# Gate logits of five dense chunks on VectorE instead of TensorE

## The reference

```python
attn = softmax(q k^T / 8, masked to 4 sink columns and a window of 128) v     # 4 x 8 heads, 768 rows, 64 wide
x = attn as (3072, 512)
h = x @ w_in                                # 512 -> 2048
y = (h * cos(h)) @ w_out                    # 2048 -> 512: the dense layer
logits = y @ w_gate + modality_bias[modality_id]      # (3072, 8)
e_idx = argmax(logits, axis=1)
gate_w = softmax(logits)[row, e_idx]
out[row] = gate_w * (relu(y[row] @ w1[e]) @ w2[e])    # e = e_idx[row]
```

## Time and profile before

| What | Value |
|---|---|
| device time, median of 3 runs | 1204.62 us (1203.62 to 1204.96) |
| span of the profiled execution | 1203.8 us |
| TensorE matmul busy | 1145.4 us (95%), 6588 instructions |
| VectorE busy | 618.9 us (51%), 1522 instructions |
| ScalarE busy | 493.6 us (41%), 1099 instructions |
| GpSimd busy | 86.7 us (7%) |
| chain that ended last | PE 86%, DVE 4%, issue 3%, DMA 3%, ACT 1% |

### The profile page before, as it was taken

The page is one execution under the profiler, slowest core; times in us unless marked ns, Lnnn a source line. Parts: engine busy times, 40 slices in busy tenths (PEclk is TensorE's granted clock), DMA queues, the critical chain, the costliest instruction groups (busy, mean ns, idle before and its releaser), DMA issues.

```text
span 1203.8 us, 20823 instructions
## 1 busy us (share of the span) xinstructions
PE 1145.4 (95%) x6588; PEld 961.5 (80%) x6589; DVE 618.9 (51%) x1522; ACT 493.6 (41%) x1099; POOL 86.7 (7%) x174
## 2 busy tenths in 40 slices
PE   6999999989999999999999999997599999999996
PEld 5777777768888888888888888886589999899895
DVE  7888888854454444444345445445773222252221
ACT  5777777753333333333334334332352221241221
POOL 0000000000000000000000000000111121221121
PEclk9999999989999999999999999998599999999998
DMA  5444444510001002002002000000573111121110
GB/s 118 143 142 142 142 142 142 173 67 1 1 9 63 1 0 70 0 0 70 0 0 70 0 0 36 1 1 35 193 257 111 35 52 36 36 105 52 35 50 18
DMA packets 33993, 76.61 MB, mean 64 GB/s; under 512 B 10398, under 2 KB 10398, under 8 KB 33952
## 3 DMA queue, kind: packets, MB, share of 16 engines
q1 hardware_dynamic: 29312, 63.50, 17.1%
q0 software_dynamic: 4640, 12.59, 3.1%
HBM read 58.77 MB, written 19.92 MB: 65 GB/s over the span
## 4 chain that ended last, share of the span: by engine, by line
PE 86%; DVE 4%; issue 3%; DMA 3%; SPq 2%; ACT 1%; POOL 0%; DVEq 0%; POOLq 0%; ACTq 0%
PE bank L1310 23%; PE bank L1324 22%; PE bank L1450 14%; PE bank L1438 12%; PE bank L1185 4%; DMA v_sink<-v_n 3%; PE bank L1219 2%; PE bank L1230 2%; PE bank L1197 2%; PE bank L1342 1%; PE bank L1420 1%; SPq L403 1%; PE bank L1411 1%; SPq L395 1%; PE bank L1187 1%
## 5 line engine op out<-in xcount | busy, mean ns | idle before, releaser
L1310 PE MATMUL bank<-x_hi,w_hi 128*128 128x512 f32 x384 | 156.1, 406 | 4.7 <-issue 4.2
L1310 PE MATMUL bank<-x_lo,w_hi 128*128 128x512 f32 x384 | 153.0, 399 | 0.0
L1310 PE MATMUL bank<-x_hi,w_lo 128*128 128x512 f32 x384 | 152.7, 398 | 0.0
L1324 PE MATMUL bank<-w_hi,g_hi 128*128 128x512 f32 x384 | 152.3, 397 | 0.4 <-DVE g_lo L986 0.4
L1324 PE MATMUL bank<-w_hi,g_lo 128*128 128x512 f32 x384 | 152.1, 396 | 0.0
L1324 PE MATMUL bank<-w_lo,g_hi 128*128 128x512 f32 x384 | 151.8, 395 | 0.0
L1145 DVE SCALAR_TENSOR_TENSOR h_lo<-bank,h_hi 128x256 fp32r<-128x256 f32 x112 | 47.6, 425 | 173.4 <-ACT h_hi L756 172.2
L1450 PE MATMUL bank<-xg_hi,w_hi 128*128 128x256 f32 x448 | 127.7, 285 | 4.3 <-DVE xg_lo L1139 2.8
L974 DVE TENSOR_SCALAR whole<-turns 128x512 f32<-128x512 f32 x96 | 41.0, 427 | 175.4 <-ACT turns L707 175.4
L1185 PE MATMUL bank<-k_sb,qz 128*128 128x256 f32 (+1 forms) x384 | 114.7, 400 | 16.8 <-DMA v_sink<-v_n 16.8
L707 ACT ACTIVATE turns<-bank 128x512 f32<-128x512 f32 x96 | 57.5, 599 | 177.7 <-PE bank L1310 177.7
(11 more groups left out here) (159 smaller groups left out, 2087.8 us busy)
## 6 DMA issues: line engine op xcount, KB each, us to landing
raw<-w_expert SPq DMA_DIRECT2D x32, 512.0 KB, 4.9
raw<-w_dense SPq DMA_DIRECT2D x16, 512.0 KB, 4.5
k_sb<-k_t SPq DMA_DIRECT2D x16, 384.0 KB, 3.3
qz<-q_t SPq DMA_DIRECT2D x32, 192.0 KB, 4.0
v_sb<-v_n SPq DMA_DIRECT2D x16, 384.0 KB, 4.4
xT_scratch<-x_stage SPq DMA_DIRECT2D x16, 384.0 KB, 4.6
x_raw<-xT_scratch SPq DMA_DIRECT2D x6, 1024.0 KB, 5.1
y_scratch<-y_sb SPq DMA_DIRECT2D x6, 1024.0 KB, 4.3
```

The lines of the kernel that those rows point to most:

```text
L1310: last = pe.matmul(H_BANK[f % 2][:, :], a[:, w], b[:, k, :], start=x == 0, stop=x == 3 * KD - 1)
L1324: last = pe.matmul(Y_BANK[t][:, :], a[f % 4][:, t * P:(t + 1) * P], b[:, w], start=f == 0 and x == 0, stop=f == FB1 - 1 and x == 2)
```

## The change

Five of the six chunks no longer send y through TensorE for their logits. The gate matrix is loaded once, transposed and flat, into all 128 partitions (`gate_rows`, 8 rows of 512 in the buffer `raw`, 2 MB in SBUF), by one DMA on SyncE's queue after `load_chunk(1)`. VectorE then makes each logit column of a tile with one `tensor_tensor_reduce`: it multiplies a tile of `y_sb` with one gate row and sums along the row. That is 4 tiles x 8 experts = 32 of them for each chunk, three in each of steps 1 to 10 of the next chunk and two in step 11: after `frac`, after `g_sb` and after `g_lo`. The product itself goes to `whole`, which is not used, so each waits for the one before. `turns`, `frac` and `cosine` become one tile. In the last four steps of the last chunk `choose_early` does the routing operations for the first 20 tiles, and after the last chunk they run over 4 tiles only. The last chunk's own turns and products are as before.

```diff
             turns = sb("turns", [P, CH], where=a)
             whole = sb("whole", [P, CH], where=a)
-            frac = sb("frac", [P, CH], where=a)
-            cosine = sb("cosine", [P, CH], where=a)
+            frac = cosine = turns
...
-        yT_sb = raw[:, 3, 0:D]
+        gate_rows = raw[:, :, :].rearrange("p a b -> p (a b)").rearrange("p (e d) -> p e d", e=NE)
...
+            load_chunk(1)
+            sp.wait_ge(w_lo_made, 2 * PIECES)
+            sp.dma_start(raw[:, :, :].rearrange("p a b -> p (a b)"), w_gate_rows.partition_broadcast(P)).then_inc(gate_rows_loaded, 16)
+            store_chunk(0)
-            with sp.Fori(1, NCH) as c:
+            with sp.Fori(2, NCH) as c:
...
-            def turn_y(c, t):
-                act.wait_ge(y_turned, CT * c + t + 1)
-                act.activation(yT_sb[:, :], TURN_BANK[:, :], ACT.Copy).then_inc(yT_made, 1)
             def copy_y(c):
                 act.wait_ge(down_done, FB1 * (c + 1))
                 act.wait_ge(y_sb_free, c + 1)
+                at_least(act, early_logits, CT * NE * c)
...
-                    if not first and f in (5, 7, 9, 11):
-                        turn_y(c - 1, (f - 5) // 2)
                     act.wait_ge(hidden_done, n + 1)
-                    at_least(act, frac_made, n)
+                    at_least(act, g_made, n)
...
+            def early_logit(c, i):
+                t, e = i // NE, i % NE
+                if i == 0:
+                    dve.wait_ge(gate_rows_loaded, 16)
...
+                at_least(dve, early_logits, CT * NE * c + i)
+                dve.tensor_tensor_reduce(out=dump[:, :], in0=y_sb[:, t, :], in1=gate_rows[:, e, :], scale=1.0, scalar=0.0,
+                                         op0=ALU.mult, op1=ALU.add,
+                                         accum_out=sums_of[:, CT * c + t, e:e + 1]).then_inc(early_logits, 1)
+            def some_logits(c, f, part):
+                i = 3 * (f - 1) + part
+                if c > 0 and 0 <= i < CT * NE:
+                    early_logit(c - 1, i)
...
+                    dve.wait_ge(frac_made, n + 1)
+                    some_logits(c, f, 0)
                     dve.wait_ge(cos_made, n + 1)
                     at_least(dve, g_lo_made, n)
                     dve.tensor_tensor(g_sb[:, :], H_BANK[f % 2][:, :], cosine[:, :], ALU.mult).then_inc(g_made, 1)
...
+                    some_logits(c, f, 1)
                     dve.wait_ge(g_hi_made, n + 1)
                     dve.tensor_tensor(g_lo[f % 4][:, :], g_sb[:, :], g_hi[f % 4][:, :].bitcast(F32), ALU.subtract).then_inc(g_lo_made, 1)
+                    some_logits(c, f, 2)
...
+                    if c == NCH - 1 and f >= FB1 - 4:
+                        choose_early(f - FB1 + 4)
...
-            with dve.Fori(1, NCH - 1) as c:
-                dense(c)
-            dense(NCH - 1, split_next=False)
+            for c in range(1, NCH):
+                dense(c, split_next=c < NCH - 1)
...
-            dve.wait_ge(logits_done, NT)
-            after(link(dve.tensor_tensor(logits[:, :, :], L_BANK[:, 0:NT * NE].rearrange("p (t e) -> p t e", e=NE),
-                                         bsel, ALU.add)))
+            late = slice(EARLY, NT)
+            few = [P, CT, NE]
+            dve.wait_ge(logits_done, CT)
+            after(link(dve.tensor_tensor(logits[:, late, :], L_BANK[:, 0:CT * NE].rearrange("p (t e) -> p t e", e=NE),
+                                         bsel[:, late, :], ALU.add)))
...
-                    if not first and f in (4, 6, 8, 10):
-                        turn_y(c - 1, (f - 4) // 2)
-                    if not first and f in (5, 7, 9, 11):
-                        route(c - 1, (f - 5) // 2)
```

More of the change, by code:

```diff
@@ L1008, in _, with choose_early @@
             full = [P, NT, NE]
+            EARLY = NT - CT
+            def choose_early(part):
+                at = slice(0, EARLY)
+                shape = [P, EARLY, NE]
+                if part == 0:
+                    dve.wait_ge(early_logits, CT * NE * (NCH - 1))
+                    after(link(dve.tensor_tensor(logits[:, at, :], sums_of[:, at, :], bsel[:, at, :], ALU.add)))
+                    link(dve.tensor_reduce(top[:, at], logits[:, at, :], AX.X, ALU.max))
+                elif part == 1:
+                    after(made[0])
+                    link(dve.tensor_tensor(weighed[:, at, :], logits[:, at, :], wide(top[:, at], shape), ALU.is_equal))
+                    link(dve.tensor_tensor(tmp[:, at, :], logits[:, at, :], wide(top[:, at], shape), ALU.subtract))
+                elif part == 2:
+                    after(made[0])
+                    after(link(dve.tensor_tensor(weighed[:, at, :], weighed[:, at, :],
+                                                 down[:, :].unsqueeze(1).broadcast_to(shape), ALU.mult)))
+                    link(dve.tensor_reduce(first_max[:, at], weighed[:, at, :], AX.X, ALU.max))
+                else:
+                    after(made[0])
+                    link(dve.tensor_tensor(onehot[:, at, :], weighed[:, at, :], wide(first_max[:, at], shape), ALU.is_equal))
+            dense(0)
             dve.wait_ge(const_loaded, 48)
@@ L1016, in _ @@
             after(n)
-            for m, x in enumerate((bsel, bpart)):
+            for m, x in enumerate((bsel[:, :, :], bpart[:, :, :])):
                 n = link(dve.tensor_tensor(x, bias_sb[:, m:m + 1, :].broadcast_to(full), wide(is_mod[:, m, :], full), ALU.mult))
             after(n)
-            after(link(dve.tensor_tensor(bsel, bsel, bpart, ALU.add)))
-            with dve.Fori(1, NCH - 1) as c:
-                dense(c)
-            dense(NCH - 1, split_next=False)
+            after(link(dve.tensor_tensor(bsel[:, :, :], bsel[:, :, :], bpart[:, :, :], ALU.add)))
+            for c in range(1, NCH):
+                dense(c, split_next=c < NCH - 1)
             dve.wait_ge(y_sb_free, NCH)
@@ L1327, in down @@
                 return last
-            def turn_y(c, t):
-                if t < 2:
-                    pe.wait_ge(y_copied_act, 2 * c + t + 1)
-                else:
-                    pe.wait_ge(y_copied_dve, 2 * c + t - 1)
-                for k in range(KD):
-                    last = pe.transpose(TURN_BANK[:, k * P:(k + 1) * P], y_sb[:, t, k * P:(k + 1) * P], ident[:, :])
-                last.then_inc(y_turned, 1)
-            def route(c, t):
-                pe.wait_ge(yT_made, CT * c + t + 1)
-                at = (CT * c + t) * NE
-                for k in range(KD):
-                    last = pe.matmul(L_BANK[:, bass.ds(at, NE)], yT_sb[:, k * P:(k + 1) * P], wg_sb[:, k, :],
-                                     start=k == 0, stop=k == KD - 1)
-                last.then_inc(logits_done, 1)
             def dense(c, last_chunk=False):
```

57 lines of the change are left out of this document (33 added, 24 removed).

## The result

| | before | changed |
|---|---|---|
| device time, median | 1204.29 us (1203.62 to 1204.96, 4 runs) | 1176.60 us (1176.14 to 1178.19, 4 runs) |
| ratio | | 0.9767 [0.9747, 0.9786] |
| span of the profiled execution | 1203.8 us | 1175.1 us |
| TensorE matmuls | x6588, 1145.4 us | x6348, 1118.3 us |
| VectorE busy | 618.9 us | 720.3 us |

2.3% faster: 1176.6 us against a forecast of 1176.8. The profiled execution itself took 1176.95 us.

The account below looks back on a forecast made before the run. TensorE, never idle in the dense layer, was taken as the bound. Removing turns and products (26.6 us) and shortening routing (1.2 us) gave 27.8 us off the 1203.8 us span, forecasting a 1176.8 us median, range 1173.5 to 1182 us.

Parts of the forecast that it names:

- TensorE's term, 26.6 us: Dense layer: removing turns (0.44 us) and products (0.89 us), 20 pairs, saves 26.6 us, at least 23.4.
- The reduce, x = 0.70 us: VectorE, dense layer: one 512-element reduce takes 0.70 us, making its step 4.6 us against TensorE's 5.6.
- Its place: Two of three reduces lie in VectorE's 0.70 us waits for ScalarE, the third in idle time behind `g_lo`; cost 0.
- Beyond it each chunk loses 31x - 34.0: Dense layer: with reduce time x over 1.10 us, `hidden` waits for `g_sb`, losing 31x - 34.0 us a chunk.
- x = 1.10 us: Dense layer: the reduce time beyond which TensorE's `hidden(13)` would wait for VectorE's `g_sb` of step 11.
- ScalarE, the DMA, the seven early operations: 0 each: ScalarE's lost copies and new wait, the 2 MB gate-row load, and `choose_early` each cost 0 on the path.
- Routing, 1.2 us: After the last chunk: seven VectorE operations on 32 instead of 192 elements save 1.2 us, bounds 0 and 1.2.
- The clock, 0 and 2.5 to either side: Behind routing: TensorE's rise from half clock may shift; taken as 0, with 2.5 us either side.
- The sum: Whole kernel: 26.6 + 1.2 = 27.8 us off the 1203.8 us span, plus 0.8 to the median, gives 1176.8 us.
- 1: Dense-layer reduces run at half rate with both sources in SBUF, x = 1.22 us; 1195.9 us; chance 0.06.
- 2: Dense-layer reduces cost two full passes, x = 1.40 us, making VectorE the bound; 1223.8 us; chance 0.03.
- 3: Dense layer: no gain, as large matmuls slow beside reduces or another wait fills the gaps; about 1204 us; chance 0.02.

Follow-up runs that it names:

- each half by itself: Changed kernel with the transposes of y, or the products with w_gate, put back on TensorE, results unused: 1188.66 us and 1198.54 us.
- all three behind `g_lo`: Changed kernel with all three reduces of a step moved behind `g_lo`, none where VectorE waits for ScalarE: 1196.61 us.
- free fourth reduce: Changed kernel with one extra reduce, result unused, in each step that has reduces: 1176.63 us.
- 5 and 6 reduces: Changed kernel with two or three extra reduces, results unused, in each step that has reduces: 1184.16 us and 1221.71 us.
- kernels of old order: The ten traced kernels with attention first in TensorE's first branch, general path behind it; their 384th large matmul starts from 352.26 to 354.19 us.
- either form: Changed kernel's reduces, or the 160 rewritten as scalar_tensor_tensor with an accumulator; the rewritten kernel took 1177.98 us.
- the exchange: Changed kernel with the sides of TensorE's first branch swapped, unused general path first, attention last: 1173.91 us.

## Why the prediction was right

- **TensorE's term, 26.6 us.** Right: 5.29 us a chunk by the windows, 26.4 for the five, and each half by itself 1.74 and 3.52 us a chunk against 1.76 and 3.56. The lower bound (23.4, if the slow matmul behind an insertion stayed) is out: the pace is 0.2335 us throughout.
- **The reduce, x = 0.70 us.** 0.686, by the row. From start to start it is 0.66 ahead of `g_sb`, and 0.80 behind `g_lo` where `whole` waits for it, instead of the 0.73 of the working. VectorE's step is 4.7 us instead of 4.6; with 0.9 us left instead of 1.0 this cost nothing. VectorE's busy time in a chunk, forecast as 66 us, is 63.8: the busy view counts overlapping instructions once.
- **Its place.** As foretold VectorE is 1.1 us late in step 3 and has caught up by step 5. That two reduces lie in ScalarE's waits was worth 18 us in the traces, 20 by the medians, as the kernel with all three behind `g_lo` shows; the prediction gave this one clause.
- **"Beyond it each chunk loses 31x - 34.0".** Right in kind (a free fourth reduce, then `hidden` waiting for `g_sb`), rough in size: 5 and 6 reduces cost the five chunks 6.2 and 44.1 us, against 5.5 and 42 by the steps as measured. It leaves out the slow matmul behind each wait. No kernel here had a reduce of another length, so the x = 1.10 us itself wasn't tried.
- **ScalarE, the DMA, the seven early operations: 0 each.** Right. The 2 MB took 11.2 us, with 88 us to spare.
- **Routing, 1.2 us.** 1.15.
- **The clock, 0 and 2.5 to either side.** Right to carry as range: of 0.8 that came back at the experts' start 0.56 is the clock, and 0.35 was lost in the products' tail. A third place was overlooked: the start of the dense layer, at half clock too, where 0.4 came back and the kernels of old order spread over 1.9 us. The upper end of the range is also added up wrongly: 3.2 (slow matmuls stay), 1.2 (no routing gain) and 2.5 (clock) over 1176.8 are 1183.7, not 1182. Nothing hangs on it here.
- **The sum.** 27.8 forecast, 28.7 of span measured, 27.7 of median. The two measured gains differ because of the execution that was profiled, not because of the kernels. Outside the span lie 1.8 to 1.9 us in every execution on record, of either kernel, where the prediction had added 0.8. So the profiled execution of the kernel before, with its 1203.8, took about 1205.6 us, 1.0 over the median; of that kernel's 23 later executions only two have a longer span (1201.5 to 1204.0, median 1202.9). The 0.8 did no harm, since it only leads from that execution back to the median: 1204.62 - 27.8 is 1176.8 as well. The mechanism and its two terms are shown. The hit to 0.2 us is luck: the clock, which was taken as 0, and the wait for the gathered rows gave 1.2 us in the profiled pair, and the median of the kernel before moves by 0.6 us from one set of runs to the next.
- **The rivals.** 1: the rate is full, in either form. 2: the mechanism exists, two to three reduces a step beyond this change. 3: the pace of the large matmuls is the same beside reduces.

## What to carry to other kernels

When the bounding engine has no idle time in a stage, small instructions taken out of it come back one for one, with the slow first matmul behind each: read their price from start to start, and give the work to an engine whose whole step, waits included, stays under the bound's. Put that work where the helper engine waits anyway; the same three instructions cost 0 in its waits and some 18 us behind them, at nearly equal busy time (720.3 and 725.8 us). Once the helper's step exceeds the bound's, the loss is the excess times the number of steps less a fixed lead: it starts suddenly and is steep. To price an effect of 1 or 2 us, compare starts round the stage that was changed; the start of another stage (here the 384th matmul, 1.9 us from the earliest to the latest) can move the whole time by as much.

## What the runs showed of the hardware that wasn't expected

- A branch of TensorE's queue took 2.89 and 3.32 us in two kernels and 0.32 to 0.34 us in the nine others at the same place of the program, and 3.6 to 4.4 us where it jumps over a whole path of the program. Which side of an `If` stands first decided when this is paid: the exchange moved it to 6.2 us and shortened the span by 3.1 us. The Trainium skill, "Runtime: NRT & Kernel Launch", section "Instruction fetch mechanics", says that a taken branch whose target has not been fetched ahead must fetch it before the program goes on. It gives no time; the long rows would fit it, but no run here shows the fetch itself.
- The view of waits put the stall at the experts' start, 4.6 us, down to VectorE's `w_lo`, on which nothing hung. Such a wait, new in a kernel whose edit lies elsewhere, is to be looked up in the engine's own queue.
- A tensor_tensor that follows a reduce without waiting for it starts 0.62 to 0.66 us after it, before its 0.69 are over and before its sum is out.
